# Attention and two expert layers on one core: pair preparation split differently, first loads in another order, 24 identity turns at the start

## The reference

```python
def _attn_ref(q, k, v, proj):              # q, k, v: (2, 8, 768, 64), proj: (64, 6)
    q_bits = (np.einsum('bhsd,dk->bhsk', q, proj) > 0)
    k_bits = (np.einsum('bhsd,dk->bhsk', k, proj) > 0)
    mask = (bucket of q_bits)[:, :, :, None] == (bucket of k_bits)[:, :, None, :]
    scores = np.where(mask, q @ k.T / sqrt(64), -1e9)
    attn = softmax(scores)
    return attn @ v
# x = attn_out as (1536, 512)
# _moe_ref:  8 experts, all rows through all, Sinkhorn-normalised gate
# _moe2_ref: 8 experts, each row through one
```

## Time and profile before

| | us |
|---|---|
| median of 3 runs (lowest to highest) | 1678.91 (1677.49 to 1680.94) |
| the profiled execution, its own time | 1673.73 |
| its span in the trace | 1672.0 |
| pairs, from the start to the last step | about 0 to 297 |
| busy over the span: PE, DVE, ACT, POOL | 94%, 37%, 28%, 20% |

### The profile page before, as it was taken

One profiled execution on the slowest core, in us unless ns is written; L12 is line 12 of the kernel. 1 busy time (PEld: TensorE's weight loads), 2 busy tenths in 40 slices (PEclk: granted clock), 3 DMA queues, 4 the chain that ended last, 5 costly groups with the idle time before them and its releaser, 6 DMA issues.

```text
span 1672.0 us, 21179 instructions
## 1 busy us (share of the span) xinstructions
PE 1567.9 (94%) x7492; PEld 1308.2 (78%) x7493; DVE 612.1 (37%) x1024; ACT 469.3 (28%) x856; POOL 336.7 (20%) x532
## 2 busy tenths in 40 slices
PE   4999999999999999999999999999999992699997
PEld 3999889788888888888888888888888871577775
DVE  5777778452211311211311311221122134554323
ACT  3677668311111111111111111111111132653113
POOL 4445543300120120030030030030030004322202
PEclk9999999999999999999999999999999995899998
DMA  5555555200110110110110020020011014754310
GB/s 133 135 155 137 139 127 163 102 1 1 51 51 1 51 50 0 50 50 0 50 50 0 4 96 0 0 100 0 0 62 39 1 51 141 264 183 141 135 40 21
DMA packets 50405, 115.94 MB, mean 69 GB/s; under 512 B 7862, under 2 KB 9910, under 8 KB 50368
## 3 DMA queue, kind: packets, MB, share of 16 engines
q1 hardware_dynamic: 44608, 102.59, 19.8%
q10 hardware_dynamic: 3360, 6.56, 1.4%
q0 software_dynamic: 2400, 6.31, 1.0%
HBM read 81.58 MB, written 13.40 MB: 57 GB/s over the span
## 4 chain that ended last, share of the span: by engine, by line
PE 84%; issue 4%; POOL 3%; DMA 3%; DVE 3%; ACT 1%; POOLq 0%; ACTq 0%; DVEq 0%; SPq 0%
PE psum L390 24%; PE psum L392 24%; PE psum L391 23%; PE psum L605 2%; DMA w_raw<-in_moe_w_dram 2%; PE psum L577 2%; PE psum L618 1%; PE psum L619 1%; PE psum L594 1%; PE psum L595 1%; PE psum L810 1%; PE psum L630 1%; POOL x_sorted L520 1%; PE psum L673 1%; DVE row_min L1100 1%
## 5 line engine op out<-in xcount | busy, mean ns | idle before, releaser
L950 ACT ACTIVATE h_hi<-psum 128x512 fp32r<-128x512 f32 x192 | 114.9, 599 | 867.3 <-PE psum L392 867.3
L390 PE MATMUL psum<-xt_lo,w_hi 128*128 128x512 f32 x768 | 303.9, 396 | 0.0
L392 PE MATMUL psum<-xt_hi,w_lo 128*128 128x512 f32 x768 | 301.1, 392 | 0.0
L390 PE MATMUL psum<-w_lo,h_hi 128*128 128x512 f32 x768 | 300.0, 391 | 0.0
L392 PE MATMUL psum<-w_hi,h_lo 128*128 128x512 f32 x768 | 299.3, 390 | 0.0
L391 PE MATMUL psum<-w_hi,h_hi 128*128 128x512 f32 x768 | 298.9, 389 | 0.0
L391 PE MATMUL psum<-xt_hi,w_hi 128*128 128x512 f32 x768 | 298.8, 389 | 0.0
L1268 DVE SCALAR_TENSOR_TENSOR h_lo<-psum,h_hi 128x512 fp32r<-128x512 f32 x192 | 132.7, 691 | 361.9 <-ACT h_hi L950 361.9
L417 POOL CAST w_hi<-w_raw 128x512 fp32r<-128x512 f32 x64 | 39.9, 624 | 813.3 <-PE psum L392 804.0
L1311 DVE SCALAR_TENSOR_TENSOR tok<-psum,route,tok 128x512 f32<-128x512 f32 x84 | 57.5, 744 | 383.8 <-PE psum L392 383.8
L392 PEld LDWEIGHTS psum<-xt_hi,w_lo 128*128 128x128 f32 x768 | 144.2, 188 | 33.4
(11 more groups left out here) (234 smaller groups left out, 1914.4 us busy)
## 6 DMA issues: line engine op xcount, KB each, us to landing
w_raw<-in_moe_w_dram SPq DMA_DIRECT2D x32, 2048.0 KB, 8.2
k_hh<-k_hi SPq DMA_DIRECT2D x32, 192.0 KB, 3.0
x_sorted<-zeros SPq DMA_DIRECT2D x21, 257.0 KB, 3.9
x_row<-x_sorted ACTq DMA_DIRECT2D x19, 256.0 KB, 2.7
k_raw<-in_k_dram SPq DMA_DIRECT2D x8, 384.0 KB, 3.3
v_raw<-in_v_dram SPq DMA_DIRECT2D x16, 192.0 KB, 3.3
k_b<-k_lo SPq DMA_DIRECT2D x16, 192.0 KB, 3.3
q_raw<-in_q_dram SPq DMA_DIRECT2D x7, 384.0 KB, 3.9
```

The costliest lines, as they stand in the source:

```text
L390: pe.matmul(acc, a[0], b[1], start=start, stop=False)
L392: return pe.matmul(acc, a[1], b[0], start=False, stop=stop)
L950: act.activation(h_s[0][:, f, :], psum[:, f % 4, :], ACT.Relu).then_inc(m1.h_hi, 1)
```

## The change

Seven edits, all in the attention stage:

- GpSimd makes `k_hi` one step earlier, in step 11 of the pair before; `split_v` moves from steps 5 and 11 to 4 and 10.
- The scaling of `q_raw` goes from GpSimd to VectorE, in step 1 (`scale_queries`).
- The semaphore for moved tiles is split into one for k and one for q; the new `k_hi` waits for the k copies of both heads alone.
- `hash_pair` does the k matmuls first and waits for q only in the middle.
- At the start k is loaded first and the second half of `proj` by ScalarE's queue; GpSimd splits `proj` between its memsets, and ScalarE places it in both weights; GpSimd waits for pair 0's split before `split_v`.
- The loads of the gate and of `tau` go to the end of SyncE's list at the start, behind the copies of the bits and the loads of pair 1; the bits of q for head 0 are moved by ScalarE's queue.
- TensorE does 24 transposes of the identity into banks 0 to 3, which nothing reads, before the first hash.

```diff
+    def move_bits(dma, u, q=True, k=True):
+
+        for wanted, dst, r, moved in ((q, q_b[u], u * D, s_q_moved[u]), (k, k_b[u], u * D + HK, s_k_moved[u])):
+            if wanted:
+                dma.dma_start(dst[HQ:HQ + 32, :].bitcast(F32), bits[r:r + 32, :].bitcast(F32)).then_inc(moved, 16)
...
+        sp.dma_start(k_raw[:], k[0]).then_inc(s_k_in, 16)
         sp.dma_start(proj_raw[0:D, :], proj).then_inc(s_proj_in, 16)
-        sp.dma_start(k_raw[:], k[0]).then_inc(s_k_in, 16)
-        sp.dma_start(proj_raw[D:P, :], proj).then_inc(s_proj_in, 16)
         for u in range(2):
             sp.dma_start(v_raw[u][:].rearrange("p t d -> p (t d)"), v_v[u]).then_inc(s_v_in[u], 16)
         sp.wait_ge(s_qk_split, 1)
         for u in range(2):
             sp.wait_ge(s_zeroed, 2 * u + 1)
             move_k(sp, u)
-        sp.dma_start(gate_raw[:], gate_in).then_inc(s_setup_dma, 16)
-        sp.dma_start(one_col[:, 0:1], tau.partition_broadcast(P)).then_inc(s_setup_dma, 16)
+        sp.wait_ge(s_bits, 2)
+        move_bits(sp, 0, q=False)
         sp.wait_ge(s_zeroed, 4)
-        sp.wait_ge(s_bits, 2)
-        move_bits(sp, 0)
         move_bits(sp, 1)
         load_pair(1)
         load_v(2, 0)
+        sp.dma_start(gate_raw[:], gate_in).then_inc(s_setup_dma, 16)
+        sp.dma_start(one_col[:, 0:1], tau.partition_broadcast(P)).then_inc(s_setup_dma, 16)
...
+            if u == 0:
+                pool.wait_ge(s_proj_in, 32)
+                pool.tensor_copy(proj_s[0][:], proj_raw[:]).then_inc(s_proj_split, 1)
+                pool.wait_ge(s_proj_split, 1)
+                pool.tensor_tensor(proj_s[1][:], proj_raw[:], proj_s[0][:].bitcast(F32),
+                                   ALU.subtract).then_inc(s_proj_split, 1)
...
         def split_qk(i, r):
 
             lower, upper = slice(0, HALF), slice(HALF, S)
-            if r == 0:
+            if r == -1:
                 for u in range(2):
-                    pool.wait_ge(s_moved[u], 128 * i)
+                    pool.wait_ge(s_k_moved[u], 64 * i)
                 pool.wait_ge(s_k_in, 16 * i + 16)
                 copy(k_hi[:], k_raw[:]).then_inc(s_qk_hi, 1)
+            if r == 0:
                 pool.wait_ge(s_qk_hi, 2 * i + 1)
                 pool.tensor_tensor(k_lo[:, lower], k_raw[:, lower], k_hi[:, lower].bitcast(F32), ALU.subtract)
             if r == 1:
                 pool.tensor_tensor(k_lo[:, upper], k_raw[:, upper], k_hi[:, upper].bitcast(F32),
                                    ALU.subtract).then_inc(s_qk_split, 1)
-                pool.wait_ge(s_q_in, 16 * i + 16)
-                pool.sem_inc(s_pool_go, 1)
-                pool.tensor_scalar(q_raw[:], q_raw[:], -SCALE, None, ALU.mult).then_inc(s_q_scaled, 1)
             if r == 2:
+                for u in range(2):
+                    pool.wait_ge(s_q_moved[u], 64 * i)
                 pool.wait_ge(s_q_scaled, i)
                 copy(q_hi[:], q_raw[:]).then_inc(s_qk_hi, 1)
                 pool.wait_ge(s_qk_hi, 2 * i + 2)
...
-            i, r = divmod(kk, 2 * IT)
-            if r < 4 and known(it, 2 * IT * (it + i + 1)):
-                split_qk(it + i + 1, r)
-            if kk % IT == IT - 1 and known(it, g + 1):
+            i, r = divmod(kk + 1, 2 * IT)
+            if at_first(g):
+                split_qk(1, -1)
+            if r < 5 and known(it, 2 * IT * (it + i + 1)):
+                split_qk(it + i + 1, r - 1)
+            if kk % IT == IT - 2 and known(it, g + 2):
                 i, u = divmod(kk // IT + 1, 2)
                 split_v(it + i, u, first=isinstance(g, int) and g < IT)
 
+        pool.wait_ge(s_qk_split, 2)
...
+        pe.wait_ge(s_ident, 1)
+        for i in range(24):
+            pe.transpose(psum[:, i % 4, 0:P], ident[:], ident[:])
         pe.wait_ge(s_ident, 3)
         pe.wait_ge(s_setup, 1)
 
         def hash_pair(i, half, bank):
 
+            first = half == 0 and isinstance(i, int) and i == 0
             if half == 0:
-                pe.wait_ge(s_qk_split, 2 * i + 2)
-                if isinstance(i, int) and i == 0:
+                pe.wait_ge(s_qk_split, 2 * i + 1)
+                if first:
                     pe.wait_ge(s_k_proj, 8)
             a = slice(half * HALF, (half + 1) * HALF)
-            for w, parts in ((proj_w[0], (q_lo, q_hi)), (proj_w[1], (k_lo, k_hi))):
+            for w, parts in ((proj_w[1], (k_lo, k_hi)), (proj_w[0], (q_lo, q_hi))):
+                if w is proj_w[0] and half == 0:
+                    pe.wait_ge(s_qk_split, 2 * i + 2)
+                    if first:
+                        pe.wait_ge(s_q_proj, 8)
                 for part in (1, 0):
                     for src in parts:
                         mm = pe.matmul(psum[:, bank, 0:HALF], w[part][:], src[:, a],
-                                       start=(w is proj_w[0] and part == 1 and src is q_lo),
-                                       stop=(w is proj_w[1] and part == 0 and src is k_hi))
+                                       start=(w is proj_w[1] and part == 1 and src is k_lo),
+                                       stop=(w is proj_w[0] and part == 0 and src is q_hi))
             mm.then_inc(s_proj, 1)
 
...
+        act.dma_start(proj_raw[D:P, :], proj).then_inc(s_proj_in, 16)
...
+        act.wait_ge(s_proj_split, 2)
+        act.wait_ge(s_proj_zeroed, 1)
+        for w_parts, at_bits, placed in ((proj_w[1], HK, s_k_proj), (proj_w[0], 0, s_q_proj)):
+            for u in range(2):
+                rows = slice(u * D, u * D + D)
+                for c, sign in ((u * D + at_bits, -1.0), (u * D + at_bits + BITS, 1.0)):
+                    for w, part in zip(w_parts, proj_s):
+                        act.activation(w[rows, c:c + BITS], part[rows, :].bitcast(F32), ACT.Copy,
+                                       scale=sign).then_inc(placed, 1)
...
+        act.wait_ge(s_bits, 2)
+        move_bits(act, 0, k=False)
...
+        dve.sem_inc(s_proj_zeroed, 1)
...
-        for u in range(2):
-            rows = slice(u * D, u * D + D)
-            for c, sign in ((u * D, -1.0), (u * D + R, 1.0)):
-                for w, part in zip(proj_w[0], proj_s):
-                    link(dve.tensor_scalar(w[rows, c:c + R], part[rows, :].bitcast(F32), sign, None, ALU.mult))
...
+        def scale_queries(i):
+            dve.wait_ge(s_q_in, 16 * i + 16)
+            dve.tensor_scalar(q_raw[:], q_raw[:], -SCALE, None, ALU.mult).then_inc(s_q_scaled, 1)
...
+            i, r = divmod(kk, 2 * IT)
+            if r == 1 and known(it, 2 * IT * (it + i + 1)):
+                scale_queries(it + i + 1)
```

30 lines of the change are left out of this document (10 added, 20 removed).

## The result

| | before | changed |
|---|---|---|
| median of 4 runs each, side by side (lowest to highest), us | 1679.28 (1677.49 to 1680.94) | 1658.74 (1657.15 to 1661.63) |
| ratio, 95% interval | | 0.988 (0.9862 to 0.9898) |
| the profiled execution; its span | 1673.73; 1672.0 | 1657.15; 1655.4 |

The account below looks back on a forecast made before the run. TensorE, 94% busy, was taken as the bound, leaving its idle time and clock to win. Pairs -9.8, first pair -1.8, clock -2.9 and start +2.0 gave -12.5 us, so 1666.4 from median 1678.91; 8-in-10 range 1660 to 1673.

Parts of the forecast that it names:

- floor of a pair: Attention pairs: undisturbed, a pair takes four triples of 7.00 us plus hash matmuls, 30.8 us, against 33.58 before.
- offset from profile to median: Whole kernel: the profiled execution lies 5.2 us below the median of runs, so 1661.2 becomes 1666.4.
- The wait for q: Hash in each pair: TensorE still waits 0.6 us for q, costing 0.75 with the matmul not overlapped.
- stall of the low parts: Steps 1 and 2 of a pair: VectorE's added scaling delays the low parts, stalling TensorE 0.3 us, 0.4 with drained pipeline.
- The clock in the pairs: Attention pairs: the two clock falls behind the wait for q go, gaining 2.9 us.
- The rival (they still fall at short stalls): Pairs: the clock still falls, there or elsewhere, at two short stalls; +2.9 us, 1669.3, chance 0.15.
- The first pair and the start: First pair gains 1.8 us; the start loses 2.0, as the moved gate load delays the first minimum to about 24.4.
- The third tile's slow clock: Start: after 4 us idle, TensorE's third tile of scores and first turns run at 1.2 GHz, costing about 1.4 us.
- The 24 turns: Start: the identity transposes bring the first hash to 2.4 GHz, 2.9 us instead of 4.54, gaining nothing on the path.
- The added wait in step 11: GpSimd in step 11: k_hi now waits for head 1's k copies; can be 1 us late at no cost.
- Slow scaling: Rival, pairs: VectorE's scaling takes 1.1 to 1.8 us, adding 3.9 to 8.8 us, 1670 to 1675; chance 0.13.
- The wait for q goes altogether: Rival, hash in the pairs: VectorE passes on less delay and the wait vanishes; 5 us less, 1661, chance 0.10.

Follow-up runs that it names:

- e7: Changed kernel with q's scaling moved to step 0, q_hi to step 1 and both halves of q_lo to step 2; median 1652.01 us.
- e4: Changed kernel with the scaling of q_raw given back to GpSimd in step 1; median 1667.57 us.
- e5: Kernel before the change, with 12 identity transposes added where TensorE waits for q; median 1673.40 us, ratio 0.9983 to before.
- e1: Changed kernel without the 24 identity transposes before the first hash; median 1659.23 us.
- e3: Changed kernel with the old start: pair edits kept, no identity transposes, old loads and old splitting of proj; median 1658.67 us.
- e6: Changed kernel with VectorE's scaling of q done twice in step 1, once into a buffer nobody then reads; median 1659.57 us.
- e8: Changed kernel with q's work one stage earlier, the gate's loads in their old place and 72 more identity transposes before the first scores; median 1652.29 us.
- e10: Changed kernel with q hashed first again, waiting for all of q_lo before the hash; median 1665.65 us.
- e2: Changed kernel with the loads of the gate and tau back in their old place on SyncE's queue; median 1656.97 us.
- e9: Changed kernel with q's work one stage earlier and the loads of the gate and tau in their old place; median 1651.17 us.
- e11: The changed kernel run again, unchanged, as a control; median 1659.29 us.
- e12: Changed kernel with k_hi back in step 0 and split_v back in steps 5 and 11; median 1661.26 us.

## Why the prediction missed

The measured 1658.7 lies 7.7 us below the forecast of 1666.4. Two steps of the prediction failed. Its floor of a pair, with the stall added on top, was mis-sized, and this is most of the first part: the traces differ by 16.6 us where 12.5 was forecast (4.1 us). The offset from profile to median was wrong, and this is the second: the 5.2 us that I added to come from the profiled execution to the median are 1.6 for the changed kernel (3.6 us).

**The floor, 30.8 us a pair, was mis-sized.** It is four times the 7.00 us of the earlier trace rows, and that triple is not like the others. TensorE's windows of the triple ahead of it, of this one and of the one behind it, in the kernel before:

```profile
113.83:120.62 6.79, 6.79 (x49) 1.00 0.53 174
120.62:127.62 7.00, 7.00 (x49) 1.00 0.89 187
127.62:134.54 6.92, 6.92 (x49) 1.00 0.38 129
```

By their mean the floor is 4 x 6.90 + 2.80 = 30.4, 0.4 lower. The rows were in the trace; I took one triple for four. The triples differ in their first step: the scores follow their turns after 0.57 us in step 6, 0.68 in step 0 and 0.77 in step 9. In step 0 they start 0.14 us behind the end of the same step's exp, as the scores of step 3 do in every kernel. In step 9 they start 0.1 later than that, and the trace has this for the weight load ahead of them:

```profile
PEld psum L594 <- issue: 0.2, 1, 0.2
```

These scores also wait for the copies of a new head (`t == 0`), but so do those of step 3, which follow after 0.63 us in e7 and 0.69 in e4; so what holds up step 9 is not shown. In every kernel with changed pairs it is 0.87 there instead of 0.77, 0.1 us a pair that the forecast did not have; one more semaphore is waited for since the split, but no run takes the split back alone.

**The wait for q was right, the stall of the low parts in part.** Step 4 takes 4.18 us and step 5, with the same work on TensorE, 3.45: the wait for q costs 0.73, forecast 0.75. VectorE's scaling takes 0.53 us against 0.55. But its price for TensorE was put at 0.4, through the low parts, on top of a triple of 7.00 that already had late scores of its own. It is 0.2 (0.88 us from turns to scores against e4's 0.69), and the path is another: the low parts cost 0.05, and the rest comes through GpSimd's slower `row_scale` and the exp.

Together, a pair takes 31.43, not 31.95. Three of the four triples of the changed kernel take 6.92, 6.79 and 7.08 us where 21.00 was forecast for the three (0.2 us), and steps 3 to 5 take 10.62 where 7.00 + 2.80 + 0.4 + 0.75 = 10.95 was (0.3 us). Six pairs gain 13.0, not 9.8: 3.2 of the 4.1 us. e7, which has no wait for q, takes 30.61 and so confirms that 30.8 is no floor.

**The clock in the pairs: right.** Forecast 2.9 for two falls, measured 1.46 and about 1.3, and e5 speaks for it that they hang on the wait for q. The size is one trace's, and e5's median has it between 0.5 and 5 us. The clock is low from 175.16 and from 243.42 on, so it fell inside the two waits and not just behind them. The rival (they still fall at short stalls) did not come: the changed kernel's first wait of 1.00 us and its six of 0.45 leave PEclk at 1.00. **At the transposes: not foreseen.** The fall at 298 of the earlier trace rows did not happen after the last pair here; the 32 transposes take 3.71 us instead of 5.38, and this brings 1.2 us. Why the clock held here was not settled: before them stands the same wait (1.28 us for VectorE's `tok`) in both. It is nothing that the change brings for sure, since the clock falls there in e1, e3, e4, e5, e6, e8 and e10 and holds in e2, e7, e9, e11 and e12.

**The first pair and the start: right, with luck in the clock's part.** -0.2 forecast (1.8 against 2.0), -0.2 measured. The first pair alone can be read from e5 and e3, which have the old start and both a slow third tile: the hash's first half ends at 43.59 and 41.64, a gain of 1.95. The first minimum was put at 24.4 and comes at 24.49. The third tile's slow clock came as told, but e3 and e5 have it with the old start too. e5's start is that of the kernel before, and its q hash comes at 42.07 instead of 40.96; so 1.1 us of the start's loss hang on which execution of before one compares with. e3 shows the start as a whole to be worth nothing in the medians.

**The 24 turns: right.** They lift the clock of the hash, which gains nothing on the path: what e1 loses lies within the scatter. The Trainium skill, "TensorE: Matmul & The Clock Gate", says in its section on the transpose mode that such turns do not count for the clock. e1's 0.52 against 0.33 us shows that they do.

**The added wait in step 11: right.** `k_hi` does not wait there; it costs nothing.

**Slow scaling: the case in the first pair alone (1.27 us), and its slope was right.** I reckoned that VectorE passes on each us. e6 measures 0.46 for 0.53. e12 shows where the slow scaling lives: next to GpSimd's `k_lo`. That the changed kernel's scaling misses it in six pairs was not forecast, so this part was luck.

**The wait for q goes altogether** did not happen, but would have been this kernel's next step: e7 does it and wins another 7 us.

**The offset of 5.2 us was wrong.** It assumed that the profiled execution is faster than the runs by something that stays. But executions scatter: from the first expert matmul to the end the traces of these kernels, all alike there, take between 1368.3 us (e11) and 1373.8 (e5). Added up from the records of the granted clock, it is low for 63 us in the expert stages of the changed kernel's trace and for 70 in e5's; but e3 has 68.5 with 1369.5 us and e12 60 with 1370.3, so the clock is at most a part of the scatter, and the rest stays open. A single profile says little about the level of the median, and here it stood at the fast end while three runs stood at the slow one.

What each pair edit is worth, taken back alone: the scaling's engine 1.24 us, the order of the hash 0.68, `k_hi` a step earlier 0.50. Together 2.42, against 2.15 for all at once; they do not add up, and this was not followed further.

## What to carry to other kernels

A floor read from one undisturbed stretch holds only for stretches of its kind: measure several, and ask what differs where they do. When a helper engine's work delays both a buffer and the small operations behind it, move it to an engine with a short form of it, but look for what the other engines do in the same moment. A load that nobody needs yet still must not move behind a backlog if an engine's list holds a wait for it ahead of work that is needed.

## What the runs showed of the chip

- VectorE's scaling of 128x768 fp32 took 0.53 us where GpSimd did only a small `row_scale` meanwhile, and 0.99 to 1.27 where GpSimd was at a two-source `k_lo` (e12 in every pair, the changed kernel in the first). GpSimd's `row_scale` took 0.43 us beside the scaling (changed), 0.62 where both began together (e7), and 0.23 without.
- A run of 24 transposes, with nothing else on TensorE, brought the hash from 0.52 to 0.33 us a matmul (e1 against the changed kernel).
- Waits of 1.65 us on TensorE, in the kernel before, came with a fall of the clock in two of seven pairs; one of 1.69 us and six of 1.14 (e10), and one of 1.00 and six of 0.45 us (changed), with none.
- The same start left the third tile of scores at 2.4 GHz in one execution (before) and at 1.2 GHz in another (e5), and the q hash 1.1 us later.
